# Weight rows right behind the chosen expert, row flags before the next keys, third keys turned behind the first dense tile

## The chip, the cores and the metric

The kernel runs on one core of one Trainium2 chip. Five engines work side by side, each on its own list of instructions: TensorE (PE, matmuls and transposes through it), VectorE (DVE), ScalarE (ACT), GpSimd (POOL, here above all the issuer of indirect transfers) and SyncE (SP, plain transfers). They wait for each other through semaphores. The metric is the device time of one execution in microseconds.

## The reference

Three parts follow each other, each on the output of the one before:

```
# 1: attention, B=2 H=8 S=768 D=64: a window of |i-j| < 16, and 24 block summaries
scores_l = scale * q @ k.T, masked to |i-j| < 16;  scores_s = scale * q @ blockmax(k).T + log(32)
x = softmax(concat(scores_l, scores_s)) @ concat(v, blockmean(v))   -> (1536, 512)
# 2: mixture of experts, E=8, capacity 1536/8 = 192 tokens each
order = argsort(-(x @ w_gate).flatten())        # all (token, expert) pairs, best first
for idx in order: give the token to the expert, if the token is free and the expert not full
out[mask] = relu(x[mask] @ w1[e]) @ w2[e]       # F = 1024
# 3: dense, D=512 -> 1024 -> 512
h = x @ w_in;  s = h * softmax(h);  out = layernorm(s) * g_ln @ w_out
```

The assignment in part 2 is greedy over all 12288 scores. What the kernel computes must give the same assignment.

## The kernel before, in words

Part 1 runs in 48 units of 128 queries and one pair of heads, and ends at about 110 us. Its instructions are not touched.

Part 2 runs in rounds, and round r finds one expert and its 192 tokens, r = 0 to 6 (the last expert gets what is left). `key` holds each token's score if it would now go to this expert, `spread_keys` writes it 16-fold into `key_wide`. TensorE turns this in 12 transposes (`turn_keys`) into three PSUM banks, ScalarE copies them to `keys` (`empty_keys`, counted by `keys_copied`). VectorE searches the 192nd best key per expert in eight passes of 4 bits (`search`, L1257 to L1267), a pass some 2.6 us. The cut goes over TensorE (`cuts`), and `close_expert` picks the expert that fills first, marks its members and takes their ranks from TensorE (`member_ranks`). `slots` gives each member a place, `choose_next` makes the next `key`, `weight_rows` writes the row numbers of the expert's weights (`widx`), `slot_flags` writes 12 tables of flags (L1332), from which TensorE counts out the token rows (`row_numbers`), and `token_rows` puts these where GpSimd reads them. GpSimd then gathers w1, the tokens and w2 of the expert, in this order, and each gather brings its part in two transfers, all on one queue.

Stage r computes expert r: `tokens` turns the gathered tokens, `hidden` (L958) and `product` (L975, in four quarters of 16 instructions) are its two matmuls, in f32. Behind the product, tiles of part 3 are computed as their rows become complete: `dense_in`, softmax and norm on VectorE and ScalarE, `dense_out`, three tiles for two stages. Stage 0 has `dense_in(0)` and stage 1 the norm of tile 0. The dense matmuls use operands split in a high and a low part. The low part of the expert's output, `yT_lo`, is VectorE's (`split_y`, L1356) after ScalarE has written the high one.

The order on every engine is written out by hand. There is no scheduler. In each stage, TensorE's search work for a later round lies between parts of the product. `WARM` = 15 filler matmuls (L1049, 30 instructions) stand before the first tokens.

In stage 1, VectorE runs, for round 2 (`round_in_odd_stage`): wait for the keys, `search(0)`, `search(1)`, then `hidden_max(0)`, the maximum of dense tile 0. ScalarE runs, after stage 0's product:

```
for n in tiles_after(r):
    if n >= 1:
        empty_turned(n - 1)
    hidden_exp(n)                     # waits for hneg, the maximum from VectorE
    if n == tiles_after(r)[-1] and r + 1 < E:
        empty_tokens(r + 1)           # copies the next expert's turned tokens
```

`empty_tokens(1)` is what the hidden product of stage 1 waits for.

## Time and profile before

| what | value |
|---|---|
| median of three runs | 523.34 us (519.41, 525.12, 523.34) |
| profiled execution | 520.79 us, its span 519.0 us |
| busy: PE, DVE, ACT, POOL | 88%, 67%, 31%, 28% |
| chain that ended last | PE 77%, DVE 9%, issue 6%, ACT 3%, DMA 2% |
| granted clock of PE, mean | 0.949 |
| weight gathers, issue to landing | 5.4 / 7.6 / 9.3 us (least, median, most) |

The profile shows one execution. A share in the chain is time in which that engine's work, or a wait for it, set the end. A row of the timeline gives the start from the span's start, the length, engine, line, operation and operands; "x12" merges twelve instructions in a row, and the bracket at its end gives the engine's idle time before it and what ended it. Instructions on PE overlap a little, so their lengths add up to slightly more than the time they take. The program's names for operands follow memory and not use: `shared` is one large buffer that holds queries, tokens and flags at different times, `w_sb` stands for both weight buffers, `psum` for all PSUM banks. The granted clock is what TensorE was given: 1.00 is 2.4 GHz and 0.50 is 1.2 GHz.

### The profile page before, as it was taken

To read this page: it belongs to the slowest core of one execution; us is meant where nothing else is said; L and a number is where in the kernel's file an instruction comes from. 1 tells how busy PE (TensorE), PEld (TensorE's weight loads), DVE (VectorE), ACT (ScalarE), POOL (GpSimd) and SP (SyncE) were. 2 spreads that over 40 slices of the span, in tenths; PEclk is the share of its full clock that TensorE was granted. 3 is DMA by queue.
4 is the path that set the end of the run, shared out by engine and by line. 5 is a ranking of instruction groups with operands and counts; after the bars stand their busy time and mean duration, and the time that the engine had idled before them with its cause. 6 is when DMAs were issued, how large, how long until landed. Compare 5 with 4: busy or idle time off the path is not lost.

```text
span 519.0 us, 8512 instructions
## 1 busy us (share of the span) xinstructions
PE 458.1 (88%) x2824; PEld 404.4 (78%) x2824; DVE 350.1 (67%) x1121; ACT 162.8 (31%) x422; POOL 144.3 (28%) x201
## 2 busy tenths in 40 slices
PE   4999899960079979999999999999998999999992
PEld 2788788860068969987997987899897889899771
DVE  4777877778889689689769878977976530400340
ACT  2777677730011132123213213311411241231330
POOL 3697677920040040041112112113102323010001
PEclk9999999976559998999999999999999999999997
DMA  9967675110054081064036008105403709000001
GB/s 255 331 229 245 204 223 154 42 32 1 0 190 165 2 283 72 0 218 158 21 141 215 20 20 307 51 21 192 163 22 124 251 21 353 2 20 1 0 22 40
DMA packets 25603, 62.45 MB, mean 120 GB/s; under 512 B 6624, under 2 KB 14176, under 8 KB 21472
## 3 DMA queue, kind: packets, MB, share of 16 engines
q0 software_dynamic: 6592, 39.85, 21.2%
q1 hardware_dynamic: 18112, 21.13, 12.6%
q10 hardware_dynamic: 864, 1.02, 0.8%
q8 instruction: 20, 0.33, 0.2%
q14 instruction: 15, 0.12, 0.1%
HBM read 55.70 MB, written 6.29 MB: 119 GB/s over the span
## 4 chain that ended last, share of the span: by engine, by line
PE 77%; DVE 9%; issue 6%; ACT 3%; DMA 2%; SPq 1%; POOL 0%; ACTq 0%; DVEq 0%; POOLq 0%
PE psum L958 17%; PE psum L975 15%; PE psum L802 5%; PE psum L1018 5%; PE psum L1025 4%; PE psum L1019 4%; PE psum L827 3%; PE psum L811 3%; PE psum L995 3%; DVE key_wide L1257 3%; PE psum L996 3%; PE psum L1000 3%; PE psum L854 2%; PE psum L1049 2%; PE psum L824 2%
## 5 line engine op out<-in xcount | busy, mean ns | idle before, releaser
L1257 DVE TENSOR_SCALAR_CACHE_REDUCE key_wide<-keys,thr 128x1536 bf16<-128x1536 f32 x49 | 88.6, 1809 | 1.0
L958 PE MATMUL psum<-shared,w_sb 128*128 128x192 f32 x512 | 87.1, 332 | 1.1 <-ACT shared L708 1.1
L958 PEld LDWEIGHTS psum<-shared,w_sb 128*128 128x128 f32 x512 | 85.9, 194 | 1.9 <-issue 1.4
L975 PE MATMUL psum<-xs,w_sb 128*128 128x192 f32 x512 | 87.0, 328 | 0.0
L975 PEld LDWEIGHTS psum<-xs,w_sb 128*128 128x128 f32 x512 | 83.0, 190 | 0.0
L596 POOL DMA_INDIRECT w_sb<-w,widx x32 | 31.1, 972 | 161.5 <-DVE widx L1328 114.2
L802 PE MATMUL psum<-w_sb,shared 128*128 128x376 f32 x96 | 43.1, 535 | 6.5 <-DMA w_sb<-k_win 6.5
L1356 DVE TENSOR_TENSOR yT_lo<-psum,yT_hi 128x384 fp32r<-128x384 f32 x16 | 8.9, 556 | 57.4 <-ACT yT_hi L708 57.4
L620 POOL TENSOR_TENSOR gain<-spread,cst 128x1 f32<-128x1 f32 x12 | 6.8, 568 | 145.6 <-DVE spread L1389 145.6
L671 ACT ACTIVATE keys<-keys,nmax 128x184 f32<-128x184 f32 x96 | 41.8, 438 | 5.7 <-DVE nmax L1141 5.2
L1141 DVE CUSTOM_DVE_ANT_0 keys<-psum,w_sb 128x184 f32<-128x184 f32 x96 | 29.7, 346 | 19.7 <-PE psum L802 15.8
L1018 PE MATMUL psum<-wout_hi,turned_hi 128*128 128x512 f32 x96 | 38.5, 401 | 4.2 <-ACT turned_hi L708 4.2
L995 PE MATMUL psum<-win_hi,yT_hi 128*128 128x512 f32 x96 | 38.5, 401 | 0.0
L1019 PE MATMUL psum<-wout_lo,turned_hi 128*128 128x512 f32 x96 | 37.6, 391 | 0.0
L996 PE MATMUL psum<-win_lo,yT_hi 128*128 128x512 f32 x96 | 37.4, 390 | 0.0
L708 ACT ACTIVATE xs<-psum 128x384 f32<-128x384 f32 x32 | 15.7, 492 | 61.0 <-PE psum L958 61.0
L708 ACT ACTIVATE yT_hi<-psum 128x384 fp32r<-128x384 f32 x16 | 7.9, 492 | 78.7 <-PE psum L975 78.7
L708 ACT ACTIVATE turned_hi<-psum 128x512 fp32r<-128x512 f32 x24 | 13.3, 595 | 61.4 <-PE psum L1010 40.9
L679 ACT ACTIVATE key_wide<-psum 128x384 f32<-128x384 f32 x48 | 23.6, 491 | 25.4 <-PE psum L811 25.2
L811 PEld LDWEIGHTS psum<-cst,keys 128*128 128x128 f32 x144 | 18.8, 145 | 12.3 <-issue 7.6
L827 PE MATMUL psum<-shared,key_wide 128*128 128x64 f32 x192 | 27.0, 263 | 0.0
L1369 DVE TENSOR_REDUCE hneg<-psum 128x1 f32<-128x1024 f32 x12 | 14.7, 1221 | 16.8 <-PE psum L1000 16.6
(146 smaller groups left out, 833.5 us busy)
## 6 DMA issues: line engine op xcount, KB each, us to landing
shared<-kT SPq DMA_DIRECT2D x8, 384.0 KB, 5.3
shared<-vT SPq DMA_DIRECT2D x8, 384.0 KB, 6.0
shared<-v_main SPq DMA_DIRECT2D x8, 384.0 KB, 3.0
x_rows<-xs SPq DMA_DIRECT2D x8, 384.0 KB, 4.2
shared<-qT SPq DMA_DIRECT2D x7, 384.0 KB, 4.7
w_sb<-w_in SPq DMA_DIRECT2D x4, 512.0 KB, 5.2
w_sb<-w_out SPq DMA_DIRECT2D x8, 256.0 KB, 4.0
shared<-v_tail SPq DMA_DIRECT2D x16, 48.0 KB, 3.2
```

The costliest lines, as they stand in the source:

```text
L671: act.activation(prob[:, s, HEAD1 * hh:HEAD1 * hh + COLS], neg[:, s, hh, :], ACT.Exp, bias=nmax[:, s, hh:hh + 1], scale=-1.0, accum_out=de ...
L708: return act.activation(dst, src, func).then_inc(unit_emptied, 1)
L802: pe.matmul(score[s][:, 0:SCOLS], q_sb[:, b, t * P:(t + 1) * P], kwin[b][:, t, :], start=True, stop=True).then_inc(scores_ready, 1)
L811: mm = pe.transpose(turn[s][:, a * P:(a + 1) * P], prob[:, s, first:first + P], ident)
L827: mm = pe.matmul(o[:, cols], probT[:, s, 2 * hh, :], vm_sb[:, b, t, cols], start=False, stop=(hh == 1))
L958: mm = pe.matmul(turn[u % 2][:, i * CAP:(i + 1) * CAP], w1_sb[:, par, first:first + P], xT[:, c, :], start=(c == 0), stop=(c == KC - 1))
L975: mm = pe.matmul(turn[u % 2][:, (d % 2) * CAP:(d % 2 + 1) * CAP], w2_sb[:, par, first:first + P], hT[:, c, :], start=(c == 0), stop=(c == ...
L995: pe.matmul(out_cols, yT_hi[:, c, tile], win_hi[:, c, cols], start=(c == 0), stop=False)
L996: pe.matmul(out_cols, yT_hi[:, c, tile], win_lo[:, c, cols], start=False, stop=False)
L1018: pe.matmul(pv[:, :], turned_hi[:, c, :], wout_hi[:, c, :], start=(c == 0), stop=False)
L1019: pe.matmul(pv[:, :], turned_hi[:, c, :], wout_lo[:, c, :], start=False, stop=False)
L1257: link(dve.tensor_scalar(hits, keys[:, :], cand, -float(CAP), ALU.is_ge, ALU.add, accum_out=count[:, :]))
```

## The change

The line numbers on the left side are those of the profile. Five things are done.

- `weight_rows(r)` moves into `close_expert(r)`, in every round, ahead of the members. For the last expert it moves ahead of `hidden_max`.
- In rounds 0 and 1 `slot_flags` comes ahead of `choose_next`, and `token_rows` ahead of `spread_keys`.
- `turn_keys(2)` leaves the end of the product of stage 0 and comes behind `dense_in(0)`, ahead of `tokens(1)`. Its three blocks use banks 2 and 3 alone (`key_bank`), so the third waits until the first is copied.
- `row_numbers(0)` comes ahead of `turn_keys(1)`; in stage 0 `cuts(1)` and `member_ranks(1)` come one quarter of the product later.
- The 15 fillers become 6 ahead of `turn_keys(0)`, 3 ahead of `row_numbers(0)` and 2 ahead of `tokens(0)`.

```diff
-WARM = 15
+WARM_TURN, WARM_ROWS, WARM_TOKENS = 6, 3, 2
...
         def key_bank(r, c):
 
+            if r == 2:
+                return bank[2 + c % 2]
...
                 for c in range(KEY_UNITS):
+                    if r == 2 and c == 2:
+                        pe.wait_ge(keys_copied, KEY_UNITS * r + 1)
                     pe.wait_ge(keys_ready, KEY_UNITS * r + c + 1)
...
-                turned_keys = KEY_UNITS * min(r + 3, ROUNDS)
+                turned_keys = KEY_UNITS * min(r + 3, ROUNDS) if n else 2 * KEY_UNITS
...
-                    pe.wait_ge(keys_copied, turned_keys - (KEY_UNITS - 1 - half if n == tiles_begun(r) else 0))
+                    pe.wait_ge(keys_copied, turned_keys - (KEY_UNITS - 1 - half if n and n == tiles_begun(r) else 0))
...
+            def warm(count):
+
+                for i in range(count):
+                    pe.matmul(pv[:, 0:2 * P], ones_f, slots_f, start=True, stop=True)
+
             pe.wait_ge(consts_ready, 1)
+            warm(WARM_TURN)
             turn_keys(0)
             cuts(0)
             member_ranks(0)
+            warm(WARM_ROWS)
+            row_numbers(0)
             turn_keys(1)
-            row_numbers(0)
             pe.wait_ge(win_lo_ready, 2 * KC)
             pe.wait_ge(wout_lo_ready, 2 * FC)
-            for i in range(WARM):
-                pe.matmul(pv[:, 0:2 * P], ones_f, slots_f, start=True, stop=True)
+            warm(WARM_TOKENS)
             tokens(0)
...
                 product(r, 0)
-                if r == 0:
-                    cuts_of(r + 1)
...
                 product(r, 1)
                 if r == 0:
-                    ranks_of(r + 1)
+                    cuts_of(r + 1)
...
-                if r % 2:
+                if r % 2 or r == 0:
                     ranks_of(r + 1)
                 product(r, 3)
-                if turns_keys(r, 3):
+                if r and turns_keys(r, 3):
                     turn_keys(r + 2)
...
                 if r == 0:
+                    turn_keys(2)
                     tokens(1)
...
                 link(dve.tensor_scalar(full[:, :], fullw[:, :], fullm[:, :], None, ALU.is_equal))
+                weight_rows(r)
                 for k, op in enumerate((ALU.is_gt, ALU.is_equal)):
...
             slots(0)
+            slot_flags(0)
             choose_next()
+            token_rows(0)
             spread_keys()
-            weight_rows(0)
-            slot_flags(0)
-            token_rows(0)
...
             slots(1)
-            choose_next()
-            spread_keys()
-            weight_rows(1)
             slot_flags(1)
             split_y(0, 1)
+            choose_next()
+            token_rows(1)
+            spread_keys()
...
-                token_rows(r - 1)
+                if r > 2:
+                    token_rows(r - 1)
```

TensorE between the end of attention and the first expert, before (L905 turns keys, L912 cuts, L918 and L919 ranks, L931 row numbers, L1049 filler, L943 turns tokens, L958 hidden product):

```order
L905 MATMUL psum<-cst,key_wide 128x128 x12
L912 MATMUL psum<-texp,cst 128x8
L918 MATMUL psum<-before,ones_b 128x26
L919 MATMUL psum<-memb,tri_b 128x2x12
L905 MATMUL psum<-cst,key_wide 128x128 x12
L931 MATMUL psum<-token_b,shared 128x2 x12
L931 MATMUL psum<-token_b,shared 64x2 x12
L1049 MATMUL psum<-cst 128x256 x15
L943 MATMUL psum<-cst,shared 128x128 x4
L943 MATMUL psum<-cst,shared 128x64 x4
L958 MATMUL psum<-shared,w_sb 128x192 x32
```

One f32 matmul or transpose here is two instructions in the trace. And with the change (the lines stand 4 lower, the filler is L1047):

```order
L1047 MATMUL psum<-cst 128x256 x6
L909 MATMUL psum<-cst,key_wide 128x128 x12
L916 MATMUL psum<-texp,cst 128x8
L922 MATMUL psum<-before,ones_b 128x26
L923 MATMUL psum<-memb,tri_b 128x2x12
L1047 MATMUL psum<-cst 128x256 x3
L935 MATMUL psum<-token_b,shared 128x2 x12
L935 MATMUL psum<-token_b,shared 64x2 x12
L909 MATMUL psum<-cst,key_wide 128x128 x12
L1047 MATMUL psum<-cst 128x256 x2
L947 MATMUL psum<-cst,shared 128x128 x4
L947 MATMUL psum<-cst,shared 128x64 x4
```

The row numbers have passed the second key turning, and the fillers stand in three places instead of one.

VectorE from the slots of round 0 to the search of round 1, before (L1314 to L1318 choose the next keys, L1241 spreads them, L1322 and L1328 are the weight rows, L1332 the flags, L1347 and L1348 the token rows):

```order
L1314 SCALAR_TENSOR_TENSOR fits<-slotv 128x12
L1315 TENSOR_TENSOR done<-done,fits 128x12
L1316 SCALAR_TENSOR_TENSOR best<-done,best 128x12
L1317 TENSOR_TENSOR behind<-rank,best 128x96
L1318 SCALAR_TENSOR_TENSOR key<-behind,logit 128x96
L1241 COPY key_wide<-key 128x512 x3
L1322 ISA wsel,wfirst<-full,cst 128x8
L1322 ISA wfirst 128x1
L1328 TENSOR_SCALAR widx<-cst,wfirst 128x2
L1332 TENSOR_SCALAR shared<-slot_b,slotv 128x192 x12
L1347 TENSOR_REDUCE sidx<-psum 64x1
L1348 TENSOR_REDUCE sidx<-psum 128x1
```

And with the change, where the weight rows (L1332 and L1338 there) have gone far ahead of this stretch and the flags are L1342:

```order
L1320 TENSOR_TENSOR slotv<-slotA,slotB 128x12
L1342 TENSOR_SCALAR shared<-slot_b,slotv 128x192 x12
L1324 SCALAR_TENSOR_TENSOR fits<-slotv 128x12
L1325 TENSOR_TENSOR done<-done,fits 128x12
L1326 SCALAR_TENSOR_TENSOR best<-done,best 128x12
L1327 TENSOR_TENSOR behind<-rank,best 128x96
L1328 SCALAR_TENSOR_TENSOR key<-behind,logit 128x96
L1357 TENSOR_REDUCE sidx<-psum 64x1
L1358 TENSOR_REDUCE sidx<-psum 128x1
L1250 COPY key_wide<-key 128x512 x3
L1266 TENSOR_SCALAR key_wide,count<-keys,cst 128x1536
L1267 SCALAR_TENSOR_TENSOR reached<-count,weigh 128x32
```

The flags have passed the choice of keys and its spreading, the token rows the spreading alone.

TensorE around dense tile 0, from the last of the product of stage 0 (L975) on, before:

```order
L975 MATMUL psum<-xs,w_sb 128x192 x16
L905 MATMUL psum<-cst,key_wide 128x128 x12
L931 MATMUL psum<-token_b,shared 128x2 x12
L931 MATMUL psum<-token_b,shared 64x2 x24
L995 MATMUL psum<-win_hi,yT_hi 128x512
L996 MATMUL psum<-win_lo,yT_hi 128x512
```

With the change the same place has no key turning in it:

```order
L979 MATMUL psum<-xs,w_sb 128x192 x8
L935 MATMUL psum<-token_b,shared 128x2 x12
L935 MATMUL psum<-token_b,shared 64x2 x24
L999 MATMUL psum<-win_hi,yT_hi 128x512
L1000 MATMUL psum<-win_lo,yT_hi 128x512
```

The key turning now stands at the end of the dense tile (L1004), ahead of the tokens of expert 1 (L947) and their hidden product (L962):

```order
L1000 MATMUL psum<-win_lo,yT_hi 128x512
L1004 MATMUL psum<-win_hi,yT_lo 128x512 x4
L909 MATMUL psum<-cst,key_wide 128x128 x12
L947 MATMUL psum<-cst,shared 128x128 x4
L947 MATMUL psum<-cst,shared 128x64 x4
L962 MATMUL psum<-shared,w_sb 128x192 x32
```

The keys of round 2 are turned behind the 24 matmuls of the dense tile, and were ahead of them.

## Rows read from the trace of the kernel before

**Rows 1.** timeline of DVE, first round's end: start us, us, instruction, operands [idle before]

```profile
140.84 0.55 DVE L1282 SCALAR_TENSOR_TENSOR member<-key,tmax,full 128x96 f32<-128x96 f32 x2
...
143.10 0.17 DVE L1314 SCALAR_TENSOR_TENSOR fits<-slotv 128x12 f32<-128x12 f32 x1
...
144.30 1.10 DVE L1241 COPY key_wide<-key 128x512 f32<-128x512 f32 x3
145.31 0.16 DVE L1322 CUSTOM_DVE_ANT_0 wsel<-full,cst 128x8 f32<-128x8 f32 x1
...
145.65 2.49 DVE L1332 TENSOR_SCALAR shared<-slot_b,slotv 128x192 bf16<-128x192 bf16 x12
149.74 0.15 DVE L1347 TENSOR_REDUCE sidx<-psum 64x1 int32<-64x2 f32 x1 [1.60 <-PE psum L931]
...
149.88 1.79 DVE L1257 TENSOR_SCALAR_CACHE_REDUCE key_wide<-keys,cst 128x1536 bf16<-128x1536 f32 x1
```

**Rows 2.** timeline of PE, first search to the end of stage 0

```profile
114.55 2.79 PE L905 MATMUL psum<-cst,key_wide 128*128 128x128 f32 x12 [3.08 <-DVE key_wide L1241]
...
142.12 0.20 PE L918 MATMUL psum<-before,ones_b 128*128 128x26 bf16 x1 [2.25 <-DVE before L1293]
...
144.88 2.79 PE L905 MATMUL psum<-cst,key_wide 128*128 128x128 f32 x12 [2.52 <-DVE key_wide L1241]
148.20 1.21 PE L931 MATMUL psum<-token_b,shared 128*128 128x2 bf16 x24 [0.53 <-DVE shared L1332]
149.33 9.70 PE L1049 MATMUL psum<-cst 128*128 128x256 f32 x30
...
160.48 10.64 PE L958 MATMUL psum<-shared,w_sb 128*128 128x192 f32 x64 [0.62 <-ACT shared L708]
170.96 2.76 PE L975 MATMUL psum<-xs,w_sb 128*128 128x192 f32 x16
173.56 0.28 PE L912 MATMUL psum<-texp,cst 128*128 128x8 f32 x2
...
181.72 1.47 PE L905 MATMUL psum<-cst,key_wide 128*128 128x128 f32 x12
```

**Rows 3.** timeline of POOL, first gather of weights (L596) and of tokens (L611)

```profile
146.84 1.29 POOL L596 DMA_INDIRECT w_sb<-w,widx  x1 [39.70 <-issue]
...
150.84 0.95 POOL L611 DMA_INDIRECT shared<-x_rows,sidx  x1 [1.46 <-DVE sidx L1348]
```

**Rows 4.** timeline of ACT, stage 1: exponentials of tile 0

```profile
191.67 1.11 ACT L745 ACTIVATE shared<-psum,hneg 128x1024 f32<-128x1024 f32 x1 [7.68 <-DVE hneg L1369]
```

**Rows 5.** chain of waits, stage 1: start us, us, what

```profile
187.17 5.43 DMA shared<-x_rows,idx_odd
```

**Rows 6.** DMA issues: the last column is us from issue to landing

```profile
out<-shared,sidx POOLq DMA_INDIRECT x12, 2.8
```

**Rows 7.** stretches: seventh figure is the granted clock (1.00 is full)

```profile
core 0: us, PE busy (x) PEld busy (x) DVE busy (x) ACT busy (x) POOL busy (x), PEclk, DMA share, GB/s
...
139.00:155.30 16.30, 10.72 (x54) 8.97 (x55) 13.14 (x52) 1.79 (x3) 5.78 (x6) 0.50 0.38 142
155.50:192.80 37.30, 33.88 (x230) 31.58 (x229) 30.75 (x86) 6.53 (x13) 5.67 (x7) 1.00 0.40 142
```

**Rows 8.** timeline of PE, stage 1: token turning, hidden product, ranks

```profile
192.74 1.56 PE L943 MATMUL psum<-cst,shared 128*128 128x128 f32 x8 [2.80 <-DMA shared<-x_rows,idx_odd]
194.82 13.05 PE L958 MATMUL psum<-shared,w_sb 128*128 128x192 f32 x64 [0.52 <-ACT shared L708]
...
216.31 0.19 PE L918 MATMUL psum<-before,ones_b 128*128 128x26 bf16 x1 [0.42 <-DVE before L1293]
```

**Rows 9.** timeline of DVE, stage 1: search of round 2, maximum, idle before L1356

```profile
170.72 0.23 DVE L1271 TENSOR_SCALAR texp<-cst,thr 128x8 f32<-128x8 f32 x1
...
185.05 1.79 DVE L1257 TENSOR_SCALAR_CACHE_REDUCE key_wide<-keys,cst 128x1536 bf16<-128x1536 f32 x1
...
190.41 1.22 DVE L1369 TENSOR_REDUCE hneg<-psum 128x1 f32<-128x1024 f32 x1
...
213.63 0.56 DVE L1356 TENSOR_TENSOR yT_lo<-psum,yT_hi 128x384 fp32r<-128x384 f32 x1 [3.73 <-ACT yT_hi L708]
```

More of the change, by code:

```diff
@@ L1445, in round_in_odd_stage @@
                 split_y(r - 1, 1)
-                weight_rows(r)
                 slot_flags(r)
@@ L1475, in round_in_even_stage @@
                 split_y(r - 1, 0)
-                weight_rows(r)
                 slot_flags(r)
@@ L1487, in _ @@
             last_expert()
+            weight_rows(E - 1)
             hidden_max(n)
@@ L1490, in _ @@
             slots(E - 1)
-            weight_rows(E - 1)
             slot_flags(E - 1)
```

## The prediction

> **What bounds the kernel now.** I read the page first, then the chain of waits, then the timelines of the four engines from 110 us to 217 us, the only stretch in which the change moves more than three small instructions. After the attention part the kernel alternates between two things: VectorE searches for the cut of the next expert (eight passes over the keys), and TensorE runs expert and dense products. Only the first search stands on the path by itself. From there on TensorE should never wait.
>
> It waits in three places. The first is between the first ranks at 142.12 and the first hidden product at 160.48: 18 us with nothing in them but 2.79 us of key turning, 1.21 of row numbers, the turning of the tokens and 9.70 of filler [rows 2]. The clock there is at the half level (0.50, so 1.2 GHz) until about 155.3 and at the full level (1.00, 2.4 GHz) after it [rows 7]. The second is in stage 1: TensorE ends the dense tile at 189.94 and idles 2.80 us for the tokens of expert 1 [rows 8], whose gather took 5.43 us from issue to landing [rows 5]. The price of this idling is more than 2.80 us. The next hidden product takes 13.05 us where the one before took 10.64 [rows 2, 8]. The third is small: 0.42 us before the ranks in stage 1 [rows 8], and equally in stages 3 and 5.
>
> **The warm-up before the first keys.** Six filler products are 12 instructions. At the full clock a 192-column instruction takes 10.64/64 = 0.166 us [rows 2], so one of 256 columns 0.22, at the half clock 0.44. TensorE idles 3.08 us there and turns the keys in 2.79 us at the half level, against 1.47 at the full one [rows 2]. The filler starts at 111.47 and ends between 114.1 (full) and 116.8 (half). I take 115.5, the middle, as if the clock came up on the way, which it did during the later filler. Then turning ends at 117.0 and not 117.3. Modelled: **-0.4 us**; ends -1.3 (turning at 114.55 at the full clock) and +2.3 (116.8 + 2.79).
>
> **Round 0.** The rows of the weights cost 145.65 - 145.31 = 0.34 us of VectorE and now stand before the member marks at 140.84 instead of at 145.31 [rows 1]. So the gather of w1 starts 4.5 us earlier, at 142.4 and not 146.84 [rows 3], and all behind it on VectorE is 0.34 later. Flags: 143.44 to 145.93. Choosing the next keys takes 1.20, to 147.13. TensorE has three fillers (6 x 0.44 = 2.6 us) in the wait for the flags, then needs 1.21 for the row numbers: 147.20. The token rows were read 1.60 after the flags' end, so now at 147.53; the token gather follows 1.10 later [rows 1, 3], at 148.6 and not 150.84: 2.2 earlier.
>
> The keys are spread at 147.7 instead of 144.30, so TensorE turns them 3.4 later, 148.3 to 151.1 [rows 1, 2]. A copy of 512 columns is about half of the 1.11 us that ScalarE needs for 1024 [rows 4]. So search 1 starts at 151.7 and not 149.88: **1.8 later**, and its result, after the same 21.07 us, at 172.8 [rows 1, 9].
>
> No row shows a token gather with its weights already landed. From its second issue, 1.26 later at 149.9, I bound it by 2.8 us (the scatter of output rows [rows 6]) and 5.43 (weights in the queue ahead of it [rows 5]). I take the middle, 4.1, since w1 is now issued 6.2 us ahead and was 4.0 ahead: tokens at 154.0, ends 152.7 and 155.3. TensorE is ready at 151.1 + 4 x 0.44 = 152.8, so it waits 1.2. Turning and copying take 2.08 [rows 8]: hidden product at **156.1 in place of 160.48**. Its filler was 30 instructions and is 4.
>
> What keeps POOL back is a small matter by the row: the first weight gather, beside the flags, took 1.29 us, the token gather beside the search 0.95 [rows 3]. The Trainium skill (SBUF — State Buffer, "Who interferes with whom" and the note on DVE blocking DMA) says that a vector copy in a two-port mode locks GpSimd out until it ends. Here the token gather would start inside the spreading of the keys, and by that rule the tokens could land up to one copy, about 0.35 us, later; the trace agrees in size, 0.34 us, on one gather.
>
> Now the clock decides. If it is up, the hidden product ends at 166.6 and half of the second product at 171.8 (2 x 2.60 from 170.96 to 173.56 [rows 2]); there the cut is now asked for, and TensorE waits for 172.8. If it is down, it ends 2.4 later, the half at 174.2, with no wait: the search hides part of what the clock takes. The ranks are asked for one piece of 2.60 later. VectorE needs for them four small instructions, then 1.28 (140.84 to 142.12 [rows 1, 2]), and now 0.34 more, an estimated 2.8 in all, so 0.2 of it sticks out. One piece of 2.6 later is the end of the product, which I call E. So E is 178.3 or 179.6, before it was 181.72 [rows 2]: -3.4 or -2.1, and I take **-2.8**. Before, the clock rose at about 155.3 after TensorE had worked almost without a gap from 144.88; now it works from 148.3 to 152.8 and then waits. No row tells whether that is enough. The Trainium skill (TensorE: Matmul & The Clock Gate, "What's actually happening") says that activity releases the throttle, and at a moment that varies from run to run of the same kernel. By that rule both values of E occur, which is why I take the middle.
>
> **Stage 1, where the change gives back more.** Flags 1 now come before the choice of keys. From the ranks VectorE needs 143.10 - 142.12 = 0.98, the 0.56 of the low half and 2.4 of flags, 2.6 of it under the product: flags at E + 1.35 [rows 1, 2, 9]. That is exactly where the key turning (1.47) used to end, so the row numbers and the dense tile do not move: the tile ends at 189.94 - 181.72 = E + 8.2.
>
> Only now does TensorE turn the keys for round 2. It has two banks for three blocks, so the third waits for a copy: 0.5 + 0.6 + 0.5 + 0.6 (a third of 1.47, and a copy with its hand-over) gives keys at E + 10.4. VectorE starts search 2 there and not at 185.05 = E + 3.3: **7 us later**. What is queued behind it: the code of VectorE reads the maximum of dense tile 0 only after two passes, 190.41 - 185.05 = 5.36 later [rows 9], at E + 15.8, though the tile is ready at E + 8.2. ScalarE waits for it with the exponentials, 1.26 later and 1.2 long (1.11 and reading the sum) [rows 4, 9], and ScalarE's copy of the turned tokens of expert 1 stands behind these exponentials. Copies end at E + 19.2, and there the hidden product starts, at E + 13.1 before [rows 8]: **+6.1**. TensorE turns its tokens by about E + 10.7 and then idles some 8.5 us. The clock falls as it did; the 2.4 us that this costs are already in the time before, so 0, ends -1.0 and +1.0.
>
> The keys of round 2 being late is hidden itself: VectorE idles 3.73 us behind that search [rows 9] and loses 1 of it.
>
> **Every later round.** The 0.34 us stand before the ranks. Where TensorE already idles 0.42 for them [rows 8] they are all on the path: three stages, **+1.0**. In the other rounds the next weights start some 4 us earlier, which nothing waits for: 0, end +0.5.
>
> **Sum.** -0.4 - 2.8 + 6.1 + 1.0 = **+3.9 us**, ends +1.4 (-1.3 - 3.4 + 5.1 + 1.0) and +8.8 (+2.3 - 2.1 + 7.1 + 1.5). The profiled execution took 520.79, less than the median 523.34; the four times average 522.2. On that average 526.1; on the profiled one 524.7, on the median 527.2. I say **526**.
>
> **Rivals.**
> A, the clock: it decides in the shortened fillers, from the point where the first filler ends at the half level. Then the first search is 2.3 later and not 0.4 earlier, E gains 2.1 and not 2.8, stage 1 costs 0.5 more: +7.8, **530**. For it: the half level for 16 us before 155.3 [rows 7]. Against: the filler there did raise it. Chance 0.2.
>
> B, faster: the new wait of stage 1 doesn't hold. If the maximum were read before the passes, the tokens would decide: second issue at E + 5.5 plus 4.1 is E + 9.6, when the keys are just turned; with 2.08 of turning and copying the hidden product starts at E + 11.8, so -1.3, and without long idling no clock loss, -2.4. Sum -0.4 - 2.8 - 1.3 - 2.4 + 1.0 = -5.9, **516**. For it: idle TensorE is the largest wait there and the keys now fill it. Against: the order of VectorE and ScalarE is fixed in code. Chance 0.08.
>
> C, the change doesn't do what it says in stage 0: the tokens land as late after their issue as in stage 1, since both gathers share a queue. Tokens at 155.3, E up to 1.3 later: +5, **527**. Chance 0.12.
>
> My own forecast has 0.6. A difference of under 1%, some 5.2 us, is about what a measurement of this kernel can't tell from none. The forecast and C lie within it almost wholly, A mostly above: faster 0.08, within 0.67, slower 0.25. The range is 520 to 531: down to the sum's low end on the profiled time less a little, up to A.
>
> **What would show it.** Weight gather near 142; token gather near 148.6; hidden product 0 near 156 with E near 179. In stage 1, ScalarE's exponentials of tile 0 at E + 17, TensorE idle 8 us or more before the hidden product, the clock at half in it. Ranks preceded by some 0.76 us idle in stages 1, 3 and 5. I am wrong if VectorE's maximum isn't what ScalarE waits for, if TensorE idles under 4 us in stage 1, or if E comes at 181 or later.

## The result, and the profile after

The changed kernel takes 525.46 us (median of 20 runs, 523.23 to 528.10). The kernel before took 522.10 in 20 runs beside them. The ratio is 1.0086 with a 95% interval of 1.0058 to 1.0114, so the change costs 4.5 us (3.0 to 5.9) on some 522. One execution of the kernel before (525.12), over 1.5% above its fastest, is left out of it; the means without that one differ by 4.5 us, the medians by 3.4. The profiled execution has a span of 523.3, 4.3 more than before.

Four timelines of the kernel after, in the stretch of the rows of before. Columns: start us, us, engine, line, instruction, operands, count, and in brackets the idle time before it with what ended it. TensorE answers to [rows 2, 8]:

```profile
111.62 1.06 PE L856 MATMUL psum<-wg_sb,key_wide 128*128 128x8 f32 x8 [0.69 <-ACT key_wide L688]
112.54 2.84 PE L1047 MATMUL psum<-cst 128*128 128x256 f32 x12
115.67 1.53 PE L909 MATMUL psum<-cst,key_wide 128*128 128x128 f32 x12 [0.30 <-DVE key_wide L1250]
...
150.68 1.61 PE L1047 MATMUL psum<-cst 128*128 128x256 f32 x4
153.20 1.02 PE L947 MATMUL psum<-cst,shared 128*128 128x128 f32 x8 [0.92 <-DMA shared<-x_rows,sidx]
154.84 12.32 PE L962 MATMUL psum<-shared,w_sb 128*128 128x192 f32 x64 [0.62 <-ACT shared L710]
...
172.69 0.39 PE L916 MATMUL psum<-texp,cst 128*128 128x8 f32 x2 [0.33 <-DVE texp L1280]
...
175.74 2.85 PE L979 MATMUL psum<-xs,w_sb 128*128 128x192 f32 x16
179.41 1.20 PE L935 MATMUL psum<-token_b,shared 128*128 128x2 bf16 x36 [0.82 <-DVE shared L1342]
...
197.46 13.39 PE L962 MATMUL psum<-shared,w_sb 128*128 128x192 f32 x64 [8.51 <-ACT shared L710]
...
219.63 0.19 PE L922 MATMUL psum<-before,ones_b 128*128 128x26 bf16 x1 [0.76 <-DVE before L1303]
```

The hidden product of stage 0 starts 5.6 us earlier than before, that of stage 1 2.6 later, behind 8.51 us of idling: this is where the gain of stage 0 goes. VectorE and ScalarE show why; they answer to [rows 1, 9] and [rows 4]:

```profile
143.77 2.25 DVE L1342 TENSOR_SCALAR shared<-slot_b,slotv 128x192 bf16<-128x192 bf16 x12
...
147.39 0.15 DVE L1357 TENSOR_REDUCE sidx<-psum 64x1 int32<-64x2 f32 x1 [0.30 <-PE psum L935]
...
188.78 1.81 DVE L1266 TENSOR_SCALAR_CACHE_REDUCE key_wide<-keys,cst 128x1536 bf16<-128x1536 f32 x1 [6.47 <-ACT keys L718]
...
194.13 1.22 DVE L1379 TENSOR_REDUCE hneg<-psum 128x1 f32<-128x1024 f32 x1
...
213.39 0.23 DVE L1280 TENSOR_SCALAR texp<-cst,thr 128x8 f32<-128x8 f32 x1
```

```profile
195.39 1.11 ACT L747 ACTIVATE shared<-psum,hneg 128x1024 f32<-128x1024 f32 x1 [6.64 <-DVE hneg L1379]
...
196.50 0.86 ACT L710 ACTIVATE shared<-psum 128x512 f32<-128x512 f32 x2
```

Search 2 starts at 188.78 and no longer at 185.05. The maximum of the dense tile (194.13) stands two passes behind its start, the exponentials behind the maximum, and the token copies (the last row), for which TensorE waits, behind the exponentials. The last row of VectorE is the end of this search.

GpSimd's gathers of w1 and of the tokens in round 0, against [rows 3]:

```profile
142.71 1.27 POOL L598 DMA_INDIRECT w_sb<-w,widx  x1 [34.17 <-issue]
144.28 0.94 POOL L598 DMA_INDIRECT w_sb<-w,widx  x1 [0.31 <-issue]
...
148.49 0.95 POOL L613 DMA_INDIRECT shared<-x_rows,sidx  x1 [3.26 <-DVE sidx L1358]
149.75 0.91 POOL L615 DMA_INDIRECT shared<-x_rows,sidx  x1 [0.30 <-issue]
```

Stretches of the kernel after, against [rows 7]; the figure behind POOL's is the granted clock:

```profile
139.00:150.00 11.00, 6.70 (x43) 5.46 (x44) 8.03 (x42) 0.60 (x1) 3.42 (x4) 0.50 0.48 165
...
155.00:160.00 5.00, 5.00 (x21) 5.00 (x21) 4.72 (x11) 0.49 (x1) 0.00 (x0) 0.66 0.69 275
160.00:180.00 20.00, 18.85 (x131) 18.05 (x130) 18.40 (x59) 2.45 (x5) 1.87 (x2) 1.00 0.14 50
...
196.00:205.00 9.00, 7.54 (x30) 7.57 (x31) 8.55 (x20) 3.00 (x7) 0.58 (x1) 0.61 0.01 2
```

The clock is at half while the row numbers and the keys of round 1 are made (139 to 150), and lower again early in each of the two hidden products.

A part that the change does not touch differs too. The last matmuls ahead of part 2, those of the router (the scores of the experts, L856), start at 111.62, in the profile before at 110.24. In the attention part one stretch was at a lower clock (first row before, second after):

```profile
56.00:62.00 6.00, 6.00 (x46) 5.10 (x45) 3.90 (x23) 4.53 (x16) 3.49 (x8) 1.00 0.57 219
```

```profile
56.00:62.00 6.00, 6.00 (x34) 5.02 (x34) 2.32 (x15) 3.11 (x11) 3.48 (x8) 0.72 0.48 184
```

Over all thirteen profiled executions of this study the router matmuls start between 109.61 and 112.60 us, with the same code ahead of them. So profiles are compared below from that point on, which I call R: span less R is 408.8 before and 411.7 after, +2.9. From R, the hidden product of stage 0 starts 7.0 us earlier than before and that of stage 1 1.3 later. The ratio over many runs, whole kernels, is what decides.

### The profile page after: what moved, and what is told of

The parts are those of the page before. It is cut to its first block, busy times and chain, and to the rows that moved or that the text cites. A ratio compares the mean times of both kernels' runs of the same rounds, so it can differ in the third digit from the quotient of the medians.

```text
span 523.3 us, 8497 instructions
## 1 busy us (share of the span) xinstructions
PE 458.2 (88%) x2816; PEld 403.3 (77%) x2816; DVE 348.7 (67%) x1121; ACT 162.3 (31%) x422; POOL 144.0 (28%) x201
## 4 chain that ended last, share of the span: by engine, by line
PE 76%; DVE 15%; ACT 3%; issue 2%; DMA 1%; SPq 1%; POOL 0%; ACTq 0%; DVEq 0%; POOLq 0%
PE psum L962 14%; PE psum L979 13%; DVE key_wide L1266 6%; PE psum L804 5%; PE psum L1022 5%; PE psum L1029 4%; PE psum L999 4%; PE psum L1023 4%; PE psum L1000 4%; PE psum L1004 4%; PE psum L829 3%; PE psum L813 3%; PE psum L856 2%; PE psum L826 2%; PE psum L909 2%
## 5 line engine op out<-in xcount | busy, mean ns | idle before, releaser
L962 PE MATMUL psum<-shared,w_sb 128*128 128x192 f32 x512 | 89.1, 337 | 9.1 <-ACT shared L710 9.1
L962 PEld LDWEIGHTS psum<-shared,w_sb 128*128 128x128 f32 x512 | 87.9, 198 | 9.8 <-issue 9.3
L829 PEld LDWEIGHTS psum<-shared,key_wide 128*128 128x128 f32 x192 | 26.0, 196 | 0.0
```

Of the source, the lines that this page charges most:

```text
L829: mm = pe.matmul(o[:, cols], probT[:, s, 2 * hh, :], vm_sb[:, b, t, cols], start=False, stop=(hh == 1))
L962: mm = pe.matmul(turn[u % 2][:, i * CAP:(i + 1) * CAP], w1_sb[:, par, first:first + P], xT[:, c, :], start=(c == 0), stop=(c == KC - 1))
```

## Experiments

All ratios are to the kernel before, run on the same chip, with the 95% interval. A difference from the change is the quotient of two such ratios and uncertain by some 0.4 to 0.5%. Each kernel has one profile. E is the end of stage 0's second product, as in the prediction: 181.72 before, 178.4 in the change. It is the modelled end of the last row less 0.16, by which that end overlaps the next row's start before (176.43 + 5.45 and 181.72).

**The third keys behind the dense tile, alone** (e9): the kernel before with that one part.

```diff
 def key_bank(r, c):
+    if r == 2:
+        return bank[2 + c % 2]
 ...
-                if turns_keys(r, 3):
+                if r and turns_keys(r, 3):
                     turn_keys(r + 2)
 ...
                 if r == 0:
+                    turn_keys(2)
                     tokens(1)
```

> The kernel before with one part of the change: the third keys are turned behind dense tile 0, in banks 2 and 3. Everything else, VectorE's order and the fillers too, is as before. The flags of round 1 still hold the dense tile to the same time, so taking the keys out ahead of it gives nothing. The theory by the prediction's steps: keys copied at E + 10.4, hidden product of stage 1 at E + 19 in place of E + 13.1, the clock as low in it as before: 5.9 us slower, ratio 1.0115 (1.008 to 1.014). A rival, that the token gather behind w1 is what bounds stage 1 and the keys only fill the wait for it: the same as before.

Measured: 1.0163 (1.0121 to 1.0205), 8.5 us. TensorE and VectorE:

```profile
176.72 5.45 PE L979 MATMUL psum<-xs,w_sb 128*128 128x192 f32 x32
183.36 1.20 PE L935 MATMUL psum<-token_b,shared 128*128 128x2 bf16 x36 [1.19 <-DVE shared L1337]
184.49 0.79 PE L999 MATMUL psum<-win_hi,yT_hi 128*128 128x512 f32 x1
...
202.98 13.27 PE L962 MATMUL psum<-shared,w_sb 128*128 128x192 f32 x64 [8.52 <-ACT shared L710]
```

```profile
199.65 1.23 DVE L1374 TENSOR_REDUCE hneg<-psum 128x1 f32<-128x1024 f32 x1
```

The idle 8.5 us of the change is there with this part alone. The hidden product starts at E + 21.0 (E is 182.0), against E + 13.1 before and E + 19.0 in the change. Of the 2.0 over the change's, 0.4 is the longer wait for the flags (1.19) and 1.6 the dense tile, which begins at a lower clock here (0.79 for one instruction, before 0.50; its first half took 4.4 us, before 2.9). This is what my expectation of 5.9 us missed. This one part costs more than the whole change, so the other parts together give time back.

**The same part taken out of the change** (e1): keys of round 2 turned behind the row numbers of round 1, in three banks as before; all else as changed.

```diff
-    if r == 2:
-        return bank[2 + c % 2]
 ...
                     rows_of_round(r + 1)
+                if r == 0:
+                    turn_keys(2)
 ...
                 if r == 0:
-                    turn_keys(2)
                     tokens(1)
```

> The change with its third key turning moved ahead of dense tile 0 again (behind the row numbers of round 1, three banks), all else kept. Theory W (the new wait: late keys hold two search passes, these the maximum, this ScalarE's exponentials and its token copy): keys are copied near E + 5.5 (E is the end of stage 0's product) instead of E + 10.3, so the maximum comes near E + 11, the exponentials near E + 12.3, and the hidden product of stage 1 starts near E + 14.5 instead of E + 19.0. TensorE's idle time ahead of it falls from 8.5 to 4 us or less. About 4.5 us faster than the change, that is about equal to the kernel before. Theory F (the cost is the clock in the shortened fillers): the same time as the change, 525.5. Theory S (the late search of round 2 costs at its own end, the cut): the search still starts 2 us late, a gain of 4 to 5 us as in W, but VectorE's idle time behind the search would then be 0 in the change.

Measured: 0.998 (0.9946 to 1.0014), 1.1% below the change.

```profile
181.85 2.11 PE L905 MATMUL psum<-cst,key_wide 128*128 128x128 f32 x12 [1.19 <-DVE key_wide L1247]
...
193.90 10.64 PE L958 MATMUL psum<-shared,w_sb 128*128 128x192 f32 x64 [2.61 <-ACT shared L708]
```

The wait falls from 8.5 to 2.6 and in this profile the product runs at the full level throughout. With e9 this shows from both sides that the third keys carry the loss. The parts do not add up: put in alone the keys cost 8.5 us, taken out of the change they give back 5.5. With the flags ahead of them, TensorE waits 0.83 for the flags and 1.19 for the keys; the keys then take 2.11 and not 1.47, the first half of the dense tile 4.0 and not 2.9, and the product starts at E + 15.4 (E is 178.5), 2.3 behind before. The new order of flags and token rows was not run alone. e1, which has it, is 0.5 to 0.6% slower than e3, e7 and e11 below, which do not, at the edge of the noise (the two profiles do not show it: span less R is 405.2 in e1 and 405.3 in e3). So no run shows a gain of it.

**The maximum ahead of the passes** (e2), the premise of rival B: the change with the maximum of the dense tile taken, in round 2, ahead of the wait for the keys.

```diff
+                if r == 2:
+                    hidden_max(n)
                 keys_wait(r)
                 search(0)
                 search(1)
-                hidden_max(n)
+                if r > 2:
+                    hidden_max(n)
```

> The change with one move more: in round 2 VectorE takes the maximum of dense tile 0 before it waits for the keys and searches. Keys and search stay as late as in the change. Theory W: ScalarE's exponentials start right behind the last key copy, near E + 10.4, the token copies end near E + 12.6, and the hidden product of stage 1 starts there instead of at E + 19.0: 6.3 us less, and 0 to 2.4 us less from a shorter clock loss. 6 to 9 us faster than the change: 517 to 519, a ratio to the kernel before of about 0.990. Theory S (late search itself costs): no gain, since the search starts as late. Theory F: no gain.

Measured: 1.0067 (1.0039 to 1.0095). The expected gain did not come. TensorE and ScalarE:

```profile
191.09 5.44 PE L962 MATMUL psum<-shared,w_sb 128*128 128x192 f32 x32 [1.76 <-ACT shared L710]
201.36 8.13 PE L962 MATMUL psum<-shared,w_sb 128*128 128x192 f32 x32 [4.83 <-ACT xs L710]
```

```profile
199.78 1.06 ACT L752 ACTIVATE shared<-shared 128x1024 f32<-128x1024 f32 x1 [8.79 <-DVE shared L1392]
...
200.84 0.85 ACT L710 ACTIVATE xs<-psum 128x384 f32<-128x384 f32 x2
```

The product does start 12.3 after E (178.8): the maximum was what the start waited for. But in its middle TensorE waits 4.83 us for a copy of xs. That copy stands in ScalarE's queue behind the squares of the dense tile, and the squares wait for VectorE's gate, behind three passes of the search. After this wait the second half ran partly at the lower clock, 8.13 us for what took 5.44.

**Both waits taken away** (e6): maximum first, the gate after one pass, its spread after two (in round 2; the old order stands behind the `else`).

```diff
+                if r == 2:
+                    hidden_max(n)
+                    keys_wait(r)
+                    search(0)
+                    hidden_gate(n)
+                    search(1)
+                    hidden_spread(n)
+                    search(2)
+                    search(3)
+                else:
 ...
```

> The run with the maximum first, and the second thing that ScalarE waits for moved too: in round 2 VectorE forms the gated product of tile 0 behind one pass, not behind three. Theory of three stacked bounds: the hidden product of stage 1 starts at E + 12.3 and runs through at the full clock (10.6 us, no gap of 4.8 us in it), TensorE asks for the cut at about E + 28 and now waits there some 6 us for the search of round 2, which is as late as in the change (result near E + 34). Cut 1.5 to 2.5 us sooner than with the maximum first, 2.9 sooner than in the change: ratio to the change 0.994 to 0.997. Rival, that ScalarE's queue was the only bound: no wait at the cut, 6 to 8 us faster than the change.

Measured: 1.0076 (1.0046 to 1.0106), not told apart from the change.

```profile
190.96 10.64 PE L962 MATMUL psum<-shared,w_sb 128*128 128x192 f32 x64 [1.76 <-ACT shared L710]
...
212.81 0.60 PE L916 MATMUL psum<-texp,cst 128*128 128x8 f32 x2 [6.01 <-DVE texp L1280]
213.25 4.70 PE L979 MATMUL psum<-xs,w_sb 128*128 128x192 f32 x16
...
405.32 0.63 PE L1023 MATMUL psum<-wout_lo,turned_hi 128*128 128x512 f32 x1
```

The hidden product is now whole, early and at the full level. But TensorE waits 6.01 us for the cut, the result of the late search itself, and the 16 instructions after it take 4.70 for 2.85. Three bounds lie one behind the other, and the edit at the queue only uncovers the third. The late keys are hidden, as the prediction says, only as long as the product is later still.

A part of the gain did get through, and was lost elsewhere. From R, the cut comes 3.3 us sooner in e6 than in the change, where I expected 2.9; the ranks of stage 1 and of the stages behind it come 2.1 sooner (in e2 1.7). Then in both profiles, and in none of the other eleven, seven instructions of a `dense_out` near 405 us, which no edit touches, run at a lower clock (the last row: 0.63 for 0.39), and 1.6 us are gone. Whether that happens in most executions the runs can't tell.

**Fillers in the wait** (e5): 19 filler products behind the tokens of stage 1, so that TensorE does not idle.

```diff
                     turn_keys(2)
                     tokens(1)
+                    warm(19)
```

> The change with 19 filler products (38 instructions, some 8.1 us at the full clock) between the turned tokens and the hidden product of stage 1, inside TensorE's idle time of 8.5 us. If part of the cost is the clock that falls in this idle time: the product starts as in the change (E + 19.0) but takes 10.6 us instead of 13.4, and the cut behind it comes 2.3 to 2.8 us sooner, held at last by the search of round 2, whose result is there 2.3 us ahead of TensorE in the change. About 2.3 us faster than the change, ratio to it 0.9955. If the clock has no part in it (its fall is owed to something else): the same as the change.

Measured: 1.0035 (1.0004 to 1.0066), 0.5% below the change.

```profile
191.37 8.48 PE L1047 MATMUL psum<-cst 128*128 128x256 f32 x38
199.96 10.64 PE L962 MATMUL psum<-shared,w_sb 128*128 128x192 f32 x64
```

The fillers keep the full level, and the product takes 10.64 where it took 13.39. So of the loss in stage 1 some 2.7 us is the clock, and the 0.5% of the runs (2.6 us, give or take 2) agrees. It is no extra loss against before, where the product took 13.05 [rows 8]. In this profile stage 0 went otherwise too: its hidden product ran at the full level (10.64), came too early for the cut and waited 2.30, and 16 instructions then took 5.47 for 2.85, so that E fell 3.1 later from R than in the change. The full level bought nothing in stage 0 there, since the search held the cut (ready 61.0 us after R in both profiles).

```profile
173.03 0.60 PE L916 MATMUL psum<-texp,cst 128*128 128x8 f32 x2 [2.30 <-DVE texp L1281]
173.48 5.47 PE L979 MATMUL psum<-xs,w_sb 128*128 128x192 f32 x16
```

**Fillers back to 15 behind the keys** (e4).

```diff
-WARM_TURN, WARM_ROWS, WARM_TOKENS = 6, 3, 2
+WARM_TURN, WARM_ROWS, WARM_TOKENS = 0, 0, 15
```

> The change with the 15 fillers back in one place ahead of the first tokens. Theory W: they end near 151 + 8.5 = 159.5 at a clock that comes up on the way, the hidden product of stage 0 starts near 161 instead of 155 at the full clock (10.5 us and not 12.3), the cut no longer waits, E comes near 182.5 instead of 178.4, and the first search starts about 1 us later: about 4 to 5 us slower than the change, 530. Theory F (the shortened fillers cost more by the clock than they give): faster than the change by 2 us or more.

Measured: 1.0166 (1.0121 to 1.0211), 0.8% above the change.

```profile
152.81 7.61 PE L1047 MATMUL psum<-cst 128*128 128x256 f32 x30
160.25 0.99 PE L947 MATMUL psum<-cst,shared 128*128 128x128 f32 x8
161.86 10.64 PE L962 MATMUL psum<-shared,w_sb 128*128 128x192 f32 x64 [0.62 <-ACT shared L710]
```

Fifteen fillers end at 160.4, when the tokens of the change have long landed (153.2). They buy the full level for the product, 1.7 us, but it starts 6.6 later from R, 1.7 of it from the first search, whose keys were turned at half the clock (2.79 us for 1.53). E comes at R + 71.1 in place of R + 66.8, and these 4.3 us are about the 0.8%. Of the 1.7, 0.7 to 0.8 is not the fillers': in this profile the router matmuls, ahead of every edit, already ran at a lower clock (1.88 us for 1.06). With that taken off, the moved and shortened fillers are still a gain of the change.

**Weight rows alone** (e3): the kernel before with the rows computed as soon as the expert is known, in all rounds (the old calls are taken out).

```diff
                 link(dve.tensor_scalar(full[:, :], fullw[:, :], fullm[:, :], None, ALU.is_equal))
+                weight_rows(r)
```

> The kernel before with the weight rows moved into close_expert in all rounds, and nothing else. Theory W with the prediction's sum: ranks wait 0.34 us longer in stages 1, 3 and 5, +1.0. The filler ahead of the first tokens keeps stage 0 as it was, +0.3. In stage 1 the tokens of expert 1 no longer stand behind w1, so they land 1.5 to 2 us sooner and TensorE idles about 1 us instead of 2.8, but ScalarE is busy with the exponentials until 192.9, so the hidden product gains at most 1 us; if the short idling no longer lets the clock fall, 2.4 more. -2 to +1, ratio 0.996 to 1.002. A rival by which early weights are the gain of the change expects 4 us less.

Measured: 0.9929 (0.9897 to 0.9961), 3.7 us faster. My own range ended at 0.996; this is the number of the rival, that early weights are a gain of 4 us.

```profile
191.45 1.02 PE L943 MATMUL psum<-cst,shared 128*128 128x128 f32 x8
194.79 10.64 PE L958 MATMUL psum<-shared,w_sb 128*128 128x192 f32 x64 [2.32 <-ACT shared L708]
```

With its weights ahead, the token gather of expert 1 is no longer waited for (before 2.80 us). A wait of 2.32 for ScalarE takes its place, and this time the clock did not fall: 10.64, not 13.05. So the product starts at E + 11.6 (E is 183.2) in place of E + 13.1 and takes 2.4 less, 3.9 in all. I had not counted on both.

**Later weight rows back at their old place** (e10), the change with the early rows in rounds 0 and 1 only.

```diff
+                if r < 2:
-                weight_rows(r)
+                    weight_rows(r)
```

> The change with the weight rows of rounds 2 to 7 back at their old places, those of rounds 0 and 1 kept in close_expert. TensorE's idle time before the ranks is 0.42 us and not 0.76 in stages 1, 3 and 5: 1.0 us faster than the change, ratio to the kernel before 1.0065. Read from the trace, since 0.2% is at the edge of the intervals. If the earlier weights of the later stages served anything, the run is no faster or slower.

Measured: 1.0084 (1.0056 to 1.0112), as the change. In the profile the ranks lose their extra wait (the first row is the wait for the tokens of stage 0):

```profile
152.46 1.02 PE L947 MATMUL psum<-cst,shared 128*128 128x128 f32 x8 [1.62 <-DMA shared<-x_rows,sidx]
...
217.92 0.19 PE L922 MATMUL psum<-before,ones_b 128*128 128x26 bf16 x1 [0.42 <-DVE before L1304]
```

0.42 in place of 0.76, in three stages; span less R is 410.55, 1.1 below the change. In the runs, where I expected 1.0065, so small a gain can't be seen, so it is shown by the profile alone.

**Fewer fillers alone** (e8): the kernel before with 8 for 15.

```diff
-WARM = 15
+WARM = 8
```

> The kernel before with 8 fillers instead of 15, nothing else. The tokens of expert 0 land near 158.5 there, behind w1, when the 15 fillers end anyway: TensorE idles for them instead. Same start of the hidden product, and the clock may be lower at it: 0 to +2.5 us, ratio 1.000 to 1.005. If the fillers themselves were the bound of stage 0: 2 to 3 us faster.

Measured: 1.0006 (0.9976 to 1.0036).

```profile
159.02 1.02 PE L943 MATMUL psum<-cst,shared 128*128 128x128 f32 x8 [3.19 <-DMA shared<-x_rows,sidx]
```

The filler was not the bound of stage 0: without it TensorE waits 3.19 for the tokens, which land behind the weights. The product then takes 12.32 for 10.64, and E comes 0.8 later from R than before.

**Early weights and fewer fillers together** (e7): early weight rows in rounds 0 and 1, and 8 fillers.

```diff
+                if r < 2:
+                    weight_rows(r)
 ...
-WARM = 15
+WARM = 8
```

> The kernel before with two edits only: weight rows in close_expert for rounds 0 and 1 alone, and 8 fillers instead of 15 ahead of the first tokens. Order of flags, keys and dense tile as before. With w1 gone ahead the first tokens land near the end of 8 fillers, so the hidden product of stage 0 starts 2.5 us sooner than with the weight rows alone, and TensorE reaches the cut of round 1 just when the search has it (slack there 2.5 us in the run with the weight rows alone). No keys are late, so stage 1 keeps its length. Ranks in stages 3 and 5 wait 0.42 and not 0.76 us. 2.5 + 0.7 faster than with the weight rows alone: ratio to the kernel before 0.985 to 0.989. If the early search and not the tokens bounds stage 0, nothing is gained beyond 0.993.

Measured: 0.9923 (0.9895 to 0.9952), short of the 0.985 to 0.989 that I expected.

```profile
154.19 0.99 PE L943 MATMUL psum<-cst,shared 128*128 128x128 f32 x8
155.79 10.64 PE L958 MATMUL psum<-shared,w_sb 128*128 128x192 f32 x64 [0.62 <-ACT shared L708]
...
189.66 12.32 PE L958 MATMUL psum<-shared,w_sb 128*128 128x192 f32 x64 [2.37 <-ACT shared L708]
```

Stage 0's product starts 4.1 earlier from R than before and E comes at R + 68.5, 2.1 sooner than with the early weights alone (e3). In stage 1 the wait of 2.37 us did cost clock this time, 1.7 us. In the runs e7 is not told apart from e3, so that the shorter filler is worth anything beside early weights is not shown.

**And fillers ahead of the first keys** (e11): e7 with six filler products before the keys of round 0.

```diff
             pe.wait_ge(consts_ready, 1)
+            for i in range(6):
+                pe.matmul(pv[:, 0:2 * P], ones_f, slots_f, start=True, stop=True)
             turn_keys(0)
```

> The run with two rounds' weight rows and 8 fillers, plus the change's 6 fillers ahead of the first keys. In the profiles the change's first search starts 6.85 us after the last gate products started, the kernel's before 7.90. If the fillers did that, by turning the keys at the full clock: 1.0 us faster than without them, the ratio to the kernel before near 0.990. If it was the chance state of the clock, no difference; if the fillers end at the half clock, up to 2 us slower.

Measured: 0.9916 (0.9882 to 0.995).

```profile
114.32 1.53 PE L905 MATMUL psum<-cst,key_wide 128*128 128x128 f32 x12 [0.30 <-DVE key_wide L1243]
...
155.22 13.57 PE L958 MATMUL psum<-shared,w_sb 128*128 128x192 f32 x64 [0.52 <-ACT shared L708]
```

The first search starts at R + 6.9 in place of R + 7.9. But the filler between keys and tokens then ran at the full clock and was over early; TensorE waited 1.94 for the tokens, the clock fell, and the product took 13.57. The microsecond was given back. e3, e7 and e11 lie within each other's intervals; they are 0.7 to 0.8% faster than the kernel before and 1.6 to 1.7% faster than the change.

## Why the prediction was right

The forecast was 526 from a sum of +3.9; the median is 525.46, +0.86% or 4.5 us. The mechanism, too, is the one forecast. That the number came out within 0.6 us is in part luck: the steps below add up to less than forecast, and the runs to more than the steps. Step by step, times of the change from R where the start of the stretch matters:

- **First keys**: -0.4 forecast, -1.05 measured (search at R + 6.85, before R + 7.90). Of the three ways in which the filler could end, it was nearest to the best: 2.84 us, then the keys in 1.53, and so in all seven profiles that have these six fillers. This term was mis-sized by the choice of the middle.
- **Round 0**: -2.8 forecast for E, -3.6 measured (E from R falls by 4.7, of which 1.05 is the first keys). Weight gather forecast 142.4 and measured 142.71, token gather 148.6 and 148.49. For the landing I took 4.1 us from the second issue; here it took at most 3.45 (149.75 to 153.20), so the hidden product started at 154.84 and not 156.1. Over the six profiles with this stage 0 it took 3.16 (e5) to 4.28 (e10), so the middle was a fair guess and this profile one of the quick ones. The clock took the way between my two cases, 12.32 us for 10.64; it did so in five of the six (12.24 to 12.32), and only in e5 was it up. The wait for the cut was 0.33, as the search hides part of what the clock takes.
- **Stage 1**: +6.1 forecast, +5.9 measured. The exponentials stand at E + 17.0 (195.39), forecast E + 17; the hidden product at E + 19.0 (197.46), forecast E + 19.2; the idle time is 8.51, forecast some 8.5. Clock: 0 forecast, +0.3 measured (13.39 against 13.05). The flags came 0.4 us sooner than forecast, so the dense tile did move a little. The late search is hidden in the change, as forecast, with 2.3 us to spare (its cut ready at 213.6, asked for at 215.88), but only by the longer wait in front of it: e6 shows it as the next bound.
- **Ranks**: +1.0 forecast, +1.0 measured, three waits of 0.76 for 0.42; e10 takes them back.

These make +2.6, and span less R says +2.9. The runs say 4.5 (their medians 3.4), and 2.9 is just under the lower end of the interval. The 1.4 us between the two profiles' R would close the gap, but R moves by 3 us over executions of the same code, and its mean over the thirteen profiles is 111.6 in the seven kernels with the new order of flags (the change, e1, e2, e4, e5, e6, e10) and 110.8 in the other six, within that movement. So I can't say that the change causes it; this stays open.

The reading of GpSimd's first gather does not hold. It took 1.27 to 1.29 us in all thirteen profiles, with the flags beside it or not, and in the change the second half of the gather runs beside the flags (144.28, flags from 143.77) and takes 0.94. So the 0.34 us over the others are not the flags' doing. And the token gather, with the spreading of the keys beside it, was issued 1.10 us after the token rows were read, as before (147.39 to 148.49): the copy did not hold it back.

**The rivals.** A, the half clock after the first filler, did not occur: the keys took 1.53. Its price was not tested. B failed twice over: its wait did hold, and with its premise made true (e2) the time hardly moved, so what I had priced at 9.8 us below the forecast gave 1, not told apart from none. Its start of the product was right (E + 11.8 forecast, E + 12.3 measured), but what stands next in ScalarE's queue was missing, and behind it the search. C did not occur: 3.16 to 4.28 us in six profiles. Its 5.43 was no upper bound, though; where the weights were issued only 4.0 us ahead, as before, the same gather took up to 6.00 (e8) and 6.49 (e9).

**Where my expectations of single runs failed**, it was in two ways. In e2 I looked only at the first wait of a chain, and in e6, where the waits came as expected, I left out the clock behind the third (4.70 for 2.85). In e3, e7, e9 and e11 it was the clock, which I could not tell from the length of an idle time.

## What to carry to other kernels

When work is moved later in one queue, follow everything that stands behind the instruction that will wait, through the second and third engine: here a key turning that nothing seemed to need early held a maximum, exponentials, a copy and the product. Before paying to remove such a wait, ask which wait lies behind it. When a change is made of several parts, time each alone, and put each back out of the whole: early weights, worth 3.7 us alone, and the moved fillers, worth 0.8% inside the change, were hidden under one part that cost 8.5 us. The shorter filler alone was worth nothing (e8).

## What the runs showed of the hardware

- Idle times of nearly one length had different prices. The hidden product of stage 1 took 10.64 us after idling 2.61 (e1), 2.32 (e3) and 1.76 (e6), all at the full level, but 12.32 after 2.37 (e7) and 2.46 (e11). Where it fell, this cost 1.7 us, and 2.9 in stage 0 of e11, as much as the edits under study. The Trainium skill (TensorE: Matmul & The Clock Gate, "What's actually happening") says that the moment at which activity releases the throttle varies from run to run. The rows here are of falls and come from one profile for each kernel, so they don't show that moment. That the clock of one kernel differs from run to run does show: over the 20 runs of the change the mean granted clock was 0.939 to 0.955, and the slower runs were in the main those with the lower clock (correlation -0.8).
- In stage 0 the gather of token rows took 3.16 to 4.28 us from its second issue to the start of TensorE, which waited for it, when the gather of its weights was issued 5.8 us ahead (six profiles), and 6.00 (e8) and 6.49 us (e9) when that was issued 4.0 us ahead.
- A part of the kernel that no edit touched ended anywhere between 109.61 and 112.60 us. A single profile can't price an edit of 1 us by its span; the rows inside the stretch can.
